# Attention by pairs of heads with shared half tiles, one rounding of query and key together, and straight-line code

## The chip, the cores and the metric
The kernel runs on one core of a Trainium2 chip. The metric is the device time of one launch in microseconds, median of several runs. The core's engines work at the same time, each through its own instruction list, and wait for one another on semaphores: TensorE (PE; PEld are its weight loads), VectorE (DVE), ScalarE (ACT), GpSimd (POOL) and SyncE (SP), which here issues nearly all DMAs. SBUF is the on-chip memory of 128 partitions; matrix results land in PSUM.

## The reference
```python
def _attn_ref(q, k, v):                     # q, k, v: 4 x 8 heads x 576 x 64
    ...
    def rotate(x):
        x1, x2 = (x[..., :half], x[..., half:])
        return np.concatenate([x1 * cos - x2 * sin, x1 * sin + x2 * cos], axis=-1)
    q_rot, k_rot = (rotate(q), rotate(k))
    scores = scale * np.matmul(q_rot, k_rot.transpose(0, 1, 3, 2))
    scores = scores - np.max(scores, axis=-1, keepdims=True)
    attn = np.exp(scores)
    attn = attn / (np.sum(attn, axis=-1, keepdims=True) + 1e-09)
    return np.matmul(attn, v)

def _moe_ref(x, w_in, w_out, s, b):         # 2304 x 512, weights 512 x 2048 and 2048 x 512
    r = np.maximum(x @ w_in, 0.0)
    return (s * (r * r) + b) @ w_out

def _moe2_ref(x, w_in, w_out):
    h = x @ w_in
    return (h * (1.0 / (1.0 + np.exp(-1.702 * h)))) @ w_out
```
The output is `_moe2_ref(_moe_ref(attention, heads side by side))`, in float32.

## The kernel before
Accurate products are built of rounded ones: a float32 value is split in a high part (type fp32r) and a low part, the rest, and a product takes two or three fp32r matmuls. Transposes are float32 matmuls against the identity `id_sb`.

Attention works head by head, 32 heads of 576 rows, that is four tiles of 128 and one half tile of 64. The jobs of a head: GpSimd rotates q and k (`rotate`, L348; VectorE for head 0). TensorE transposes both together (`prep`, L520). ScalarE rounds q and k (`hi_q`, `hi_k`), VectorE makes the low parts (`lo_q`, `lo_k`), each on 64 partitions, and SP copies the two parts of K to the other 64 partitions (`copy_halves`, L388). A score job (`S_job`, L476) makes 128 rows of scores by 576 keys in four matmuls (256 and 320 columns, with K's high and low part); VectorE takes the maximum of a row (L595), ScalarE the exp with its sum (L542). A transpose job (`X_job`, L487) turns one block column of E: four transposes of 128 rows and one of 64. ScalarE rounds the result (L549), VectorE subtracts (L602), and `PV` (L496) multiplies by V, high and low part side by side, in 18 matmuls. ScalarE takes the result out of PSUM in two halves (`main_out`, `rest_out`), GpSimd adds these per pair of heads; the inverse sums are widened, transposed (`B_job`, L510), and VectorE multiplies (`finish`, L613) into `xT`.

Each engine follows an order written by hand, a list of tokens such as `S2@1`: job S, tile 2, of the head one ahead (`PE_ORDER`, L229, and the lists behind it). `steps` (L284) unrolls the first and last heads and runs the rest as a loop over pairs. `SLOTS` says which of four PSUM tiles of two banks a job uses; a job waits until its predecessor in the tile has been read (`released`, L253).

The two MLPs follow in six chunks of 384 tokens each. In a step i of 16, `H` (L720) makes 128 hidden rows (12 matmuls), ScalarE and VectorE apply the function and split it, and `Y` (L736) adds the products of step i - 2 to the output. Weights come by DMA, are split by both engines, and stay in SBUF; four of them are split before the MLP begins. The first and last chunk of each MLP are unrolled, the others a loop of two chunks (`chunks`, L683).

## Time and profile before
| | us |
|---|---|
| median of 3 runs | 1200.91 (1199.67 to 1201.15) |
| span of the profiled execution | 1201.6 |
| TensorE busy | 1157.1 |
| VectorE busy | 596.4 |
| ScalarE busy | 584.1 |
| GpSimd busy | 218.5 |

The profile is of one execution; its span goes from the first to the last instruction. The first MLP's first matmul starts at 390.54 us, so attention takes about a third of the span. The chain that ended last is to 85% TensorE, 66% of it the two lines of the MLP (L732 and L756).

### The profile page before, as it was taken

To read this page: it belongs to the slowest core of one execution; us is meant where nothing else is said; L and a number is where in the kernel's file an instruction comes from. 1 tells how busy PE (TensorE), PEld (TensorE's weight loads), DVE (VectorE), ACT (ScalarE), POOL (GpSimd) and SP (SyncE) were. 2 spreads that over 40 slices of the span, in tenths; PEclk is the share of its full clock that TensorE was granted. 3 is DMA by queue.
4 is the path that set the end of the run, shared out by engine and by line. 5 is a ranking of instruction groups with operands and counts; after the bars stand their busy time and mean duration, and the time that the engine had idled before them with its cause. 6 is when DMAs were issued, how large, how long until landed. Compare 5 with 4: busy or idle time off the path is not lost.

```text
span 1201.6 us, 19306 instructions
## 1 busy us (share of the span) xinstructions
PE 1157.1 (96%) x6576; PEld 1054.0 (88%) x6576; DVE 596.4 (50%) x954; ACT 584.1 (49%) x1146; POOL 218.5 (18%) x310
## 2 busy tenths in 40 slices
PE   3999999999998999999999999999999999999998
PEld 3777887787786999999899999999999999999997
DVE  3788888888886653333233334653332322323222
ACT  3888989989986543323222234542222222223222
POOL 5466576566541000000000000000000000000000
PEclk9999999999998999999999999999999999999999
DMA  4322232232230430000000001320000000000000
GB/s 112 83 67 65 71 75 58 68 75 65 65 86 18 130 99 2 1 1 1 2 1 1 1 1 53 123 71 1 27 1 1 27 1 26 0 26 0 27 1 27
DMA packets 66437, 46.78 MB, mean 39 GB/s; under 512 B 30672, under 2 KB 55888, under 8 KB 66384
## 3 DMA queue, kind: packets, MB, share of 16 engines
q1 hardware_dynamic: 66384, 46.03, 14.0%
q8 instruction: 38, 0.62, 0.2%
q14 instruction: 15, 0.12, 0.0%
HBM read 31.85 MB, written 4.72 MB: 30 GB/s over the span
## 4 chain that ended last, share of the span: by engine, by line
PE 85%; ACT 7%; issue 5%; DVE 2%; DMA 0%; SPq 0%; ACTq 0%; DVEq 0%
PE hps L732 33%; PE acc L756 33%; PE psum L506 7%; PE psum L483 4%; ACT E L542 4%; PE psum L493 4%; PE psum L530 2%; ACT out_rest L563 1%; ACT EThi L549 1%; PE psum L517 1%; DVE ETlo L602 1%; DVE negmax L595 1%; ACTq L43 0%; DMA Klo<-Klo 0%; DMA kraw<-in_k_dram 0%
## 5 line engine op out<-in xcount | busy, mean ns | idle before, releaser
L732 PE MATMUL hps<-xlo,Whi 128*128 128x384 f32 x768 | 257.3, 335 | 1.8 <-issue 1.8
L732 PE MATMUL hps<-xhi,Whi 128*128 128x384 f32 x768 | 257.9, 336 | 0.6 <-issue 0.6
L732 PE MATMUL hps<-xhi,Wlo 128*128 128x384 f32 x768 | 257.8, 336 | 0.0
L732 PEld LDWEIGHTS hps<-xlo,Whi 128*128 128x128 f32 x768 | 144.2, 188 | 6.2 <-issue 2.2
L732 PEld LDWEIGHTS hps<-xhi,Whi 128*128 128x128 f32 x768 | 144.4, 188 | 5.2 <-issue 0.9
L732 PEld LDWEIGHTS hps<-xhi,Wlo 128*128 128x128 f32 x768 | 144.1, 188 | 0.0
L493 PE MATMUL psum<-id_sb,E 128*128 128x128 f32 (+1 forms) x800 | 134.1, 280 | 9.9 <-ACT E L542 7.2
L595 DVE TENSOR_REDUCE negmax<-psum 128x1 f32<-128x576 f32 (+1 forms) x160 | 120.4, 754 | 42.3 <-PE psum L483 41.1
L493 PEld LDWEIGHTS psum<-id_sb,E 128*128 128x128 f32 (+1 forms) x800 | 97.2, 141 | 49.5 <-issue 27.4
L834 ACT ACTIVATE ghi<-act,sb_sb 128x384 fp32r<-128x384 f32 x96 | 59.2, 617 | 157.8 <-PE acc L756 149.5
L858 DVE SCALAR_TENSOR_TENSOR glo<-act,sb_sb,ghi 128x384 fp32r<-128x384 f32 x96 | 59.5, 619 | 145.9 <-ACT ghi L834 145.9
L756 PE MATMUL acc<-ghi,Wlo 128*128 128x384 f32 x384 | 129.0, 336 | 0.0
L861 DVE TENSOR_TENSOR glo<-act,ghi 128x384 fp32r<-128x384 f32 x96 | 53.6, 559 | 151.7 <-ACT ghi L836 151.7
L756 PE MATMUL acc<-glo,Whi 128*128 128x384 f32 x384 | 128.9, 336 | 0.0
L756 PE MATMUL acc<-ghi,Whi 128*128 128x384 f32 x384 | 128.8, 335 | 0.0
L542 ACT ACTIVATE E<-psum,negmax 128x576 f32<-128x576 f32 (+1 forms) x160 | 119.0, 744 | 16.8 <-DVE negmax L595 16.3
L836 ACT CAST ghi<-act 128x384 fp32r<-128x384 f32 x96 | 49.3, 514 | 156.7 <-PE acc L756 156.7
L483 PE MATMUL psum<-Khi,Q 128*128 128x256 f32 x320 | 104.7, 348 | 12.6 <-ACT E L542 8.8
L855 DVE TENSOR_TENSOR act<-hps,act 128x384 f32<-128x384 f32 x96 | 53.5, 558 | 124.1 <-ACT act L830 124.1
L756 PE MATMUL acc<-Wlo,ghi 128*128 128x512 f32 x288 | 113.9, 396 | 0.0
L756 PE MATMUL acc<-Whi,glo 128*128 128x512 f32 x288 | 113.7, 395 | 0.0
L756 PE MATMUL acc<-Whi,ghi 128*128 128x512 f32 x288 | 111.9, 389 | 0.0
(66 smaller groups left out, 1897.4 us busy)
## 6 DMA issues: line engine op xcount, KB each, us to landing
wraw<-in_moe_w_in_dram SPq DMA_DIRECT2D x32, 256.0 KB, 2.7
wraw<-in_moe_w_out_dram SPq DMA_DIRECT2D x32, 256.0 KB, 3.0
Khi<-Khi SPq DMA_DIRECT2D x32, 144.0 KB, 2.3
Klo<-Klo SPq DMA_DIRECT2D x32, 144.0 KB, 2.5
out_dram<-xT SPq DMA_DIRECT2D x6, 768.0 KB, 3.5
qraw<-in_q_dram SPq DMA_DIRECT2D x32, 128.0 KB, 2.2
kraw<-in_k_dram SPq DMA_DIRECT2D x32, 128.0 KB, 2.2
vraw<-in_v_dram SPq DMA_DIRECT2D x32, 128.0 KB, 2.0
```

The lines of the kernel that those rows point to most:

```text
L483: mm = pe.matmul(ps[:, C0 + a:C0 + b], Q[h.odd][:, j * P:(j + 1) * P], K[h.odd][:, a:b], start=(n == 0), stop=(n == 1))
L493: mm = pe.transpose(ps[:, a:b], E[h.odd][0:rows, t, j * P:(j + 1) * P], id_sb[0:rows, 0:rows])
L506: mm = pe.matmul(O[:, C0 + a:C0 + b], V[h.odd][:, j, :, :].rearrange("p a d -> p (a d)"), X[:, j, a:b], start=(j == 0 and n == 0), stop=(j ...
L542: act.activation(E[h.odd][0:rows, j, 0:S], row(psum_of(h, "S", j))[0:rows], ACT.Exp, bias=negmax[h.odd][0:rows, j:j + 1], accum_out=sums[h ...
L595: dve.tensor_reduce(negmax[h.odd][0:rows, j:j + 1], row(psum_of(h, "S", j))[0:rows], AX_X, ALU.max, negate=True).then_inc(max_done, 1)
L732: mm = pe.matmul(ps[:, 0:CH], w[i][:, kt * P:(kt + 1) * P], piece(x[par][:], kt), start=(kt == 0 and j == 0), stop=(kt == KT - 1 and j == 2))
L756: mm = pe.matmul(dst, lhsT, rhs, start=(i == 0 and j == 0), stop=(i == NF - 1 and j == 2))
L834: act.activation(ghi[i % 2][:], a[:], ACT.Identity, bias=sb_sb[:, 1:2]).then_inc(g_hi, 1)
L836: act.copy(ghi[i % 2][:], a[:]).then_inc(g_hi, 1)
L855: dve.tensor_tensor(a[:], hps[i % HB][:, 0:CH], a[:], ALU.mult).then_inc(g_done, 1)
L858: dve.scalar_tensor_tensor(glo[i % 2][:], a[:], sb_sb[:, 1:2], ghi[i % 2][:].bitcast(F32), ALU.add, ALU.subtract).then_inc(g_lo, 1)
L861: dve.tensor_tensor(glo[i % 2][:], a[:], ghi[i % 2][:].bitcast(F32), ALU.subtract).then_inc(g_lo, 1)
```

## The change
Attention now works pair by pair. E's half tiles of the two heads share tiles: for the second head of a pair the tokens are laid out so that its half tile comes first, and one score job (`ST`) makes the 64 tail rows of both heads at once, in ten matmuls; one transpose job (`XT`) makes both heads' tail columns. All transposes have 128 rows and 128 columns. `PV` takes 20 matmuls. Query and key are rotated in one set of instructions over both, rounded in one instruction with a scale per partition, and the low part is one instruction too; four DMAs then copy Q's parts and K's parts to their places. ScalarE copies the result of `PV` once, whole (`evac`), and a DMA brings the half that is needed on the other partitions (`load_rest`). V's high part moves from ScalarE to GpSimd, the widening of the inverse sums from ScalarE to VectorE, and `finish` has three instructions. k and v are loaded in the layout that q had. All engines' lists are straight code: a static order for 16 pairs (`program`), also for GpSimd and SP, and the MLP's loops are unrolled in the same order of steps. One weight tile is split early and two at the end of attention; each chunk's output leaves in six DMAs where one did.

```diff
-    PE_ORDER = order("X0@0 S2@1 X1@0 S3@1 X2@0 S4@1 X3@0 X4@0 "
-                     "prep@3 S0@2 PV0@0 PV1@0 B@-1 PV2@0 PV3@0 PV4@0 S1@2")
+PE_ORDER = order("PV0@-1 B@-2 X00@0 prep1@1 X01@0 X02@0 S00@1 X03@0 PV1@-1 S01@1 S02@1 X10@0 X11@0 ST@1 prep0@2 "
+                 "XT@0 S03@1 S10@1 X12@0 S11@1 X13@0 S12@1 S13@1")
+POOL_ORDER = order("add0@-2 vlo1@-1 add1@-2 V0@0 vlo0@0 rot0@2 V1@0 rot1@2")
+SP_ORDER = order("load1@0 loadv0@-1 rest1@-3 load0@1 copy0@0 copy1@0 loadv1@-1 rest0@-2")
...
+def program(toks, ops, after=None):
+    for s in range(FIRST, NPAIR + 4):
+        for kind, h, j, ahead in toks:
+            if 0 <= s + ahead < NPAIR:
+                ops[kind](s + ahead, h, j)
+        if after:
+            after(s)
...
-    def steps(eng, order, ops, after=None):
-        with eng.Fori(lo // 2, hi // 2) as pair:
-            for odd in range(2):
-                step(Head(pair, odd))
...
-    def rotate(eng, h, n, by_cos, by_sin, chain, done, before):
-        for t, by in ((cos, by_cos), (sin, by_sin)):
-            eng.tensor_tensor(by[:, :, :].rearrange("p t (a f) -> p t a f", a=2), halves,
-                              tabs[t][:, :, :].unsqueeze(2).broadcast_to([P, NT, 2, HALF]), ALU.mult).then_inc(chain, 1)
+    def rotate(eng, g, by_cos, by_sin, chain, done, count):
+        for tab, by in ((cos, by_cos), (sin, by_sin)):
+            eng.tensor_tensor(by.rearrange("p t w (a f) -> p t (w a) f", a=2), halves,
+                              tab[:, :, :].unsqueeze(2).broadcast_to([P, NT, 4, HALF]), ALU.mult).then_inc(chain, 1)
...
-        def copy_halves(h):
-            e, g = h.odd, h.g
-            need(sp, k_hi, g + 1)
-            sp.dma_start(Khi[e][0:D, :].bitcast(F32), Khi[e][D:P, :].bitcast(F32)).then_inc(copied[e], 16)
-            need(sp, k_lo, g + 1)
-            sp.dma_start(Klo[e][0:D, :].bitcast(F32), Klo[e][D:P, :].bitcast(F32)).then_inc(copied[e], 16)
+        def copies(p, h, _):
+            sp.wait_ge(qk_lo, 2 * p + h + 1)
+            need(sp, s_done, 2 * NM * (p - 1) + NM * (h + 1))
+            need(sp, sT_done, p)
+            at = h * TAIL
+            for part in range(2):
+                sp.dma_start(Q[h][rows_of(part), at:at + S].bitcast(F32), QK[h][0:D, part, :].bitcast(F32)).then_inc(copied[h], 16)
+            for half in range(2):
+                sp.dma_start(K[h][rows_of(half), :, :].bitcast(F32), QK[h][D:P, :, :].bitcast(F32)).then_inc(copied[h], 16)
...
+        def load_rest(p, h, _):
+            sp.wait_ge(evac_done, 2 * p + h + 1)
+            need(sp, added, 2 * (p - 1) + h + 1)
+            sp.dma_start(rest[rows_of(h), :], O[h][rows_of(1 - h), :]).then_inc(rest_in[h], 16)
...
+        def hi_V(p, h, _):
+            pool.wait_ge(v_in[h], 32 * (p + 1))
+            need(pool, pv_done, 2 * (p - 1) + h + 1)
+            pool.tensor_tensor(V[h][:, :, h, :], vraw[h][:], zero[:, :].unsqueeze(2).broadcast_to([P, NT, D]), ALU.add).then_inc(v_hi, 1)
...
+        def add(p, h, _):
+            pool.wait_ge(evac_done, 2 * p + h + 1)
+            pool.wait_ge(rest_in[h], 16 * (p + 1))
+            need(pool, x_done, p)
+            r = rows_of(h)
+            if h == 0:
+                pool.tensor_tensor(osum[r, :], O[0][r, :], rest[r, :], ALU.add).then_inc(added, 1)
+            else:
+                for signal in made:
+                    pool.wait_ge(signal, made[signal])
+                pool.tensor_tensor(osum[r, 0:MAIN], O[1][r, TAIL:S], rest[r, TAIL:S], ALU.add)
+                pool.tensor_tensor(osum[r, MAIN:S], O[1][r, 0:TAIL], rest[r, 0:TAIL], ALU.add).then_inc(added, 1)
...
-            for a, b in HALVES:
-                for n, K in enumerate((Khi, Klo)):
-                    mm = pe.matmul(ps[:, C0 + a:C0 + b], Q[h.odd][:, j * P:(j + 1) * P], K[h.odd][:, a:b],
-                                   start=(n == 0), stop=(n == 1))
+            for a, b, c in PIECES[h]:
+                for part in range(2):
+                    mm = pe.matmul(ps[:, a:b], Q[h][:, at:at + P], K[h][:, part, c:c + b - a], start=part == 0, stop=part == 1)
+        def ST_job(p, _, __):
+            for h in range(2):
+                pe.wait_ge(copied[h], 64 * (p + 1))
+            freed(pe, before[("ST", p, 0, 0)])
+            ps, r = banks("ST"), ROW[0]
+            tails = Q[0][:, MAIN:MAIN + P], Q[1][:, 0:P]
+            for a, b, parts in ((r, BANK, ((0, r, 0, BANK - r), (1, r, TAIL, TAIL + BANK - r))),
+                                (BANK, r + S, ((0, BANK, BANK - r, S), (1, BANK, TAIL + BANK - r, S), (1, r + MAIN, 0, TAIL)))):
+                for n, (h, at, c, d) in enumerate(parts):
+                    for part in range(2):
+                        mm = pe.matmul(ps[:, at:at + d - c], tails[h], K[h][:, part, c:d], start=n == 0 and part == 0,
+                                       stop=n == len(parts) - 1 and part == 1, skip_group_check=True)
+            mm.then_inc(sT_done, 1)
...
-            for t in range(NT):
-                rows = P if t < NT - 1 else TAIL
-                a, b = cols(t)
-                mm = pe.transpose(ps[:, a:b], E[h.odd][0:rows, t, j * P:(j + 1) * P], id_sb[0:rows, 0:rows])
+            ps, r = banks("X", h, j), ROW[0]
+            at = r + MAIN if h == 0 else r - P
+            pe.transpose(ps[:, at:at + P], ET[p % 2][:, j * P:(j + 1) * P], id_sb[:])
+            c = h * TAIL + j * P
+            for t in range(NM):
+                mm = pe.transpose(ps[:, r + t * P:r + (t + 1) * P], E[p % 2][:, t, h, c:c + P], id_sb[:])
+        def XT_job(p, _, __):
+            pe.wait_ge(exp_done, 2 * NM * (p + 1))
+            pe.wait_ge(expT_done, p + 1)
+            freed(pe, before[("XT", p, 0, 0)])
+            ps, r = banks("XT"), ROW[0]
+            pe.transpose(ps[:, r - P:r], ET[p % 2][:, S - P:S], id_sb[:])
+            pe.transpose(ps[:, r + MAIN:r + MAIN + P], ET[p % 2][:, MAIN:MAIN + P], id_sb[:])
+            for t in range(NM):
+                both = E[p % 2][:, t, :, :].rearrange("p h s -> p (h s)")[:, MAIN:MAIN + P]
...
-            for a, b in HALVES:
-                parts = (EThi, ETlo) if j < NT - 1 else (EThi,)
-                for n, X in enumerate(parts):
-                    mm = pe.matmul(O[:, C0 + a:C0 + b], V[h.odd][:, j, :, :].rearrange("p a d -> p (a d)"), X[:, j, a:b],
-                                   start=(j == 0 and n == 0), stop=(j == NT - 1))
+            shift = TAIL if h == 0 else 0
+            for j in range(NT):
+                for a, b, c in PIECES[h]:
+                    for n in range(2):
+                        if j < NM:
+                            x = (Xhi, Xlo)[n][h][:, j, c:c + b - a]
+                        else:
+                            x = (XThi, XTlo)[n][:, c + shift:c + shift + b - a]
+                        mm = pe.matmul(ps[:, a:b], V[h][:, j, :, :].rearrange("p a d -> p (a d)"), x,
+                                       start=j == 0 and n == 0, stop=j == NM and n == 1)
+            mm.then_inc(pv_done, 1)
...
-        def main_out(h, _):
-            need(act, pv_done, NT * (h.g + 1))
-            need(act, x_done, h.pair)
-            act.copy(out_main[mine(h), :], psum_of(h, "PV")[mine(h), C0:C0 + S]).then_inc(main_done, 1)
-        def rest_out(h, _):
-            need(act, pv_done, NT * (h.g + 1))
-            need(act, added, h.pair)
-            act.copy(out_rest[mine(h), :], psum_of(h, "PV")[mine(h + 1), C0:C0 + S]).then_inc(rest_done, 1)
+        def evac(p, h, _):
+            act.wait_ge(pv_done, 2 * p + h + 1)
+            need(act, added, 2 * (p - 1) + h + 1)
+            act.copy(O[h][:], row(banks("PV", h), h)).then_inc(evac_done, 1)
-        def hi_q(h, _):
-            need(act, prep_t, h.g + 1)
-            need(act, s_done, NT * (h.g - 1))
-            act.activation(Q[h.odd][0:D, 0:S], row(psum_of(h, "prep"))[0:D], ACT.Copy, scale=SCALE).then_inc(q_hi, 1)
-        def hi_k(h, _):
-            need(act, prep_t, h.g + 1)
-            need(act, s_done, NT * (h.g - 1))
-            act.copy(Khi[h.odd][D:P, :], row(psum_of(h, "prep"))[D:P]).then_inc(k_hi, 1)
+        def qk(p, h, _):
+            act.wait_ge(prep_t, 2 * p + h + 1)
+            need(act, copied[h], 64 * p)
+            act.activation(QK[h][:, 0, :], row(banks("prep", h), h), ACT.Identity, scale=qk_scale[:, 0:1]).then_inc(qk_hi, 1)
-        def lo_k(h, _):
-            need(dve, k_hi, h.g + 1)
-            dve.tensor_tensor(Klo[h.odd][D:P, :], row(psum_of(h, "prep"))[D:P], Khi[h.odd][D:P, :].bitcast(F32),
-                              ALU.subtract).then_inc(k_lo, 1)
+        def qk_low(p, h, _):
+            dve.wait_ge(qk_hi, 2 * p + h + 1)
+            dve.scalar_tensor_tensor(QK[h][:, 1, :], row(banks("prep", h), h), qk_scale[:, 0:1],
+                                     QK[h][:, 0, :].bitcast(F32), ALU.mult, ALU.subtract).then_inc(qk_lo, 1)
...
+            dve.reciprocal(inv_c[:], sums_eps[:]).then_inc(inv_step, 1)
+            dve.wait_ge(inv_step, p + 1)
+            dve.tensor_copy(inv[:], inv_c[:, 0:2 * NM].rearrange("p (h t) -> p t h", h=2).unsqueeze(3)
+                            .broadcast_to([P, NM, 2, D])).then_inc(inv_done, 1)
+        def finish_pair(p):
+            b, t = p // KT * S, p % KT
+            ps, r = banks("B"), ROW[0]
+            dve.wait_ge(b_done, p + 1)
+            dve.wait_ge(added, 2 * p + 2)
+            dve.tensor_tensor(xT[:, t, b:b + MAIN], ps[:, r:r + MAIN], osum[:, 0:MAIN], ALU.mult)
+            for h in range(2):
+                at = r + MAIN + h * TAIL
+                last = dve.tensor_tensor(xT[rows_of(h), t, b + MAIN:b + S], ps[rows_of(h), at:at + TAIL],
+                                         osum[rows_of(h), MAIN:S], ALU.mult)
+            last.then_inc(x_done, 1)
...
+    if s == NPAIR - 1:
+        eng.wait_ge(prep_t, 2 * NPAIR)
+        eng.wait_ge(v_lo, 2 * NPAIR)
+        for i in range(EARLY, AHEAD):
+            split_w(eng, i, hi)
...
-def chunks(eng, chunk):
-    for mlp in range(2):
-        first = mlp * NCH
-        chunk(first, 0, mlp)
-        with eng.Fori(0, (NCH - 2) // 2) as two:
-            for o in range(2):
-                chunk(2 * two + (first + 1 + o), (1 + o) % 2, mlp)
-        chunk(first + NCH - 1, (NCH - 1) % 2, mlp)
+        for n in range(STEPS + LAG):
+            if n < STEPS:
+                H_step(pe, n)
+            if n >= LAG:
+                Y_step(pe, n - LAG)
```

Here is TensorE's list in the loop of attention before, from the end of one score job to the next; L493 is a transpose job of E, L530 the transposes of q and k, L483 a score job, L506 `PV`:
```order
L483 MATMUL psum<-Klo,Q 128x320
L493 MATMUL psum<-id_sb,E 128x128 x4
L493 MATMUL psum<-id_sb,E 128x64
L493 MATMUL psum<-id_sb,E 128x128 x4
L493 MATMUL psum<-id_sb,E 128x64
L530 MATMUL psum<-id_sb,qkrot 128x128 x4
L530 MATMUL psum<-id_sb,qkrot 128x64
L483 MATMUL psum<-Khi,Q 128x256
L483 MATMUL psum<-Klo,Q 128x256
```
And after the change the same kind of place, behind the first `PV` of a step (L482), with the transpose jobs of E and ET (L448 and L451), those of q and k (L502 and L504) and a score job (L424):
```order
L482 MATMUL psum<-XThi,V 128x320
L482 MATMUL psum<-XTlo,V 128x320
L448 MATMUL psum<-id_sb,ET 128x128
L451 MATMUL psum<-id_sb,E 128x128 x4
L502 MATMUL psum<-id_sb,rot 128x128
L504 MATMUL psum<-id_sb,rot 128x128 x4
L448 MATMUL psum<-id_sb,ET 128x128
L451 MATMUL psum<-id_sb,E 128x128 x4
L448 MATMUL psum<-id_sb,ET 128x128
L451 MATMUL psum<-id_sb,E 128x128 x4
L424 MATMUL psum<-K,Q 128x256 x2
L424 MATMUL psum<-K,Q 128x320 x2
```
A job of one head still has five transposes, and none of them has 64 rows or columns now.

SP's queue in the loop before, for one head: the loads of q and k, the two copies of K, the load of V.
```order
L365 DMA qraw<-in_q_dram 128x4x64
L366 ISA
L366 DMA qraw<-in_q_dram 64x64
L370 DMA kraw<-in_k_dram 128x256
L371 DMA kraw<-in_k_dram 64x64
L43 REGISTER_ALU
L391 DMA Khi<-Khi 64x576
L393 DMA Klo<-Klo 64x576
L384 DMA vraw<-in_v_dram 128x256
L386 DMA vraw<-in_v_dram 64x64 x2
```
After, for the latter part of a pair (`QK` holds both rounded parts, `O` the copied result of `PV`):
```order
L329 DMA Q<-QK 64x576 x2
L331 DMA K<-QK 64x1152 x2
L329 DMA Q<-QK 64x576 x2
L331 DMA K<-QK 64x1152 x2
L320 DMA vraw<-in_v_dram 128x4x64
L321 DMA vraw<-in_v_dram 64x64
L336 DMA rest<-O 64x576
```
Four copies a head stand where two stood, and the V load of the second head stands behind all of them.

GpSimd's list before, for the first head of a pair and the rotation of the next: rotation (L354 to L360), V's low part (L447).
```order
L354 TENSOR_TENSOR byc<-kraw,kc 128x320
L354 TENSOR_TENSOR bys<-kraw,ks 128x320
L43 REGISTER_ALU
L359 TENSOR_TENSOR qkrot<-byc,bys 128x5x32
L360 TENSOR_TENSOR qkrot<-bys,byc 128x5x32
L43 ISA
L447 TENSOR_TENSOR V<-vraw,V 128x5x64
```
After, from the rounding of the second head's V on (L385 high part, L390 low part, L400 to L406 the sums of a pair):
```order
L385 TENSOR_TENSOR V<-vraw,zero 128x5x64
L301 TENSOR_TENSOR byc<-raw,cos 128x640
L301 TENSOR_TENSOR bys<-raw,sin 128x640
L306 TENSOR_TENSOR rot<-byc,bys 128x10x32
L307 TENSOR_TENSOR rot<-bys,byc 128x10x32
L400 TENSOR_TENSOR osum<-O,rest 64x576
L390 TENSOR_TENSOR V<-vraw,V 128x5x64
L405 TENSOR_TENSOR osum<-O,rest 64x512
L406 TENSOR_TENSOR osum<-O,rest 64x64
```
The rotation has half as many instructions of twice the size, V's high part is new here, and the sums stand between two rotations.

## Rows read from the trace of the kernel before

**Rows 1.** The page: busy times, and TensorE's busy tenths in 40 slices
```profile
PE 1157.1 (96%) x6576; PEld 1054.0 (88%) x6576; DVE 596.4 (50%) x954; ACT 584.1 (49%) x1146; POOL 218.5 (18%) x310
PE   3999999999998999999999999999999999999998
```
**Rows 2.** Stretches: us, busy PE PEld DVE ACT POOL (instructions), clock, DMA, GB/s
```profile
60.00:346.00 286.00, 274.45 (x1816) 225.46 (x1816) 240.00 (x375) 256.64 (x527) 180.76 (x247) 1.00 0.28 68
...
376.00:383.00 7.00, 4.89 (x33) 3.64 (x31) 3.97 (x8) 3.19 (x5) 0.00 (x0) 1.00 0.00 1
383.00:391.00 8.00, 7.61 (x33) 6.63 (x33) 2.91 (x4) 4.17 (x7) 0.00 (x0) 0.57 0.21 67
...
396.00:398.00 2.00, 2.00 (x14) 2.00 (x13) 1.68 (x3) 0.98 (x2) 0.00 (x0) 1.00 0.73 245
...
591.00:596.00 5.00, 5.00 (x22) 5.00 (x21) 0.82 (x2) 1.11 (x2) 0.00 (x0) 0.66 0.01 3
```
**Rows 3.** Timeline of TensorE: start, us, instruction; broadcasts L517, first MLP matmul L732
```profile
65.38 0.80 PE L517 MATMUL psum<-id_sb,invb 128*128 128x128 f32 x5
...
353.81 0.80 PE L517 MATMUL psum<-id_sb,invb 128*128 128x128 f32 x5
...
390.54 0.44 PE L732 MATMUL hps<-xhi,Whi 128*128 128x384 f32 x1
```
**Rows 4.** Timeline of TensorE: score and transpose jobs, a 64-row load
```profile
289.68 0.29 PE L483 MATMUL psum<-Khi,Q 128*128 128x256 f32 x1
289.81 0.28 PE L483 MATMUL psum<-Klo,Q 128*128 128x256 f32 x1
...
290.22 0.80 PE L493 MATMUL psum<-id_sb,E 128*128 128x128 f32 x5
290.95 0.39 PE L483 MATMUL psum<-Khi,Q 128*128 128x256 f32 x1
...
291.59 0.60 PE L493 MATMUL psum<-id_sb,E 128*128 128x128 f32 x4
...
350.55 0.66 PE L493 MATMUL psum<-id_sb,E 128*128 128x128 f32 x4 [0.17 <-ACT E L542]
351.14 0.13 PEld L493 LDWEIGHTS psum<-id_sb,E 64*128 64x128 f32 x1 [0.17 <-issue]
```
**Rows 5.** Groups by shape, 60 to 346 us: busy, mean ns, idle before
```profile
L493 PEld LDWEIGHTS psum<-id_sb,E 64*128 64x128 f32 x128 | 17.2, 135 | 21.4 <-issue 21.4
```
**Rows 6.** The chain that ended last, in order of time: start, us
```profile
320.27 2.38 PE psum L506 x18
...
397.05 2.08 PE acc L756 x12
```
**Rows 7.** Groups by shape, 60 to 346 us, on the other engines
```profile
L595 DVE TENSOR_REDUCE negmax<-psum 128x1 f32<-128x576 f32 x103 | 77.8, 756 | 16.4 <-PE psum L483 15.5
...
L542 ACT ACTIVATE E<-psum,negmax 128x576 f32<-128x576 f32 x102 | 76.1, 746 | 7.9 <-DVE negmax L595 7.5
...
L549 ACT CAST EThi<-psum 128x576 fp32r<-128x576 f32 x102 | 65.3, 641 | 3.1
...
L354 POOL TENSOR_TENSOR byc<-qraw,qc 128x320 f32<-128x320 f32 x26 | 22.6, 867 | 0.0
...
L452 POOL TENSOR_TENSOR out_main<-out_main,out_rest 128x576 f32<-128x576 f32 x13 | 18.3, 1410 | 0.0
```
**Rows 8.** DMA issues of the whole span: count, KB each, median us to landing
```profile
wraw<-in_moe_w_out_dram SPq DMA_DIRECT2D x32, 256.0 KB, 3.0
Khi<-Khi SPq DMA_DIRECT2D x32, 144.0 KB, 2.3
```
**Rows 9.** Timeline near the start: an issue on SP, a matmul of a score job
```profile
15.12 0.49 SPq L391 DMA_DIRECT2D Khi<-Khi  x1
...
18.72 0.41 PE L483 MATMUL psum<-Klo,Q 128*128 128x256 f32 x1
```
**Rows 10.** Timeline of TensorE at the loop's back jump in the first MLP
```profile
586.97 0.44 PE L732 MATMUL hps<-xhi,Whi 128*128 128x384 f32 x1 [0.63 <-issue]
...
590.29 0.45 PE L732 MATMUL hps<-xlo,Whi 128*128 128x384 f32 x1 [1.85 <-issue]
```

988 lines of the change are left out of this document (471 added, 517 removed).

## Prediction
> **What bounds the kernel now.** I read the page first. TensorE is busy for 96% of the span, VectorE and ScalarE for half, and TensorE's digit is 9 in nearly all of the 40 slices [rows 1]. So the time is TensorE's; an edit pays only by its matmuls, its waits or its clock. Next the table of stretches. In steady attention (60 to 346 us) TensorE is busy 274.5 of 286 us, ScalarE 256.6, VectorE 240.0 and GpSimd 180.8, at a granted clock of 1.00 [rows 2]. The broadcast transposes of pair 0 and pair 13 start at 65.38 and 353.81 us [rows 3]: 288.4 us for 13 pairs, 22.2 us a pair, of which 21.3 are TensorE work (96% [rows 2]) and 0.9 waits. The MLP runs from 390.54 us [rows 3] to the end, 811.1 us.
>
> What a reader should find is what these 21.3 us consist of. A score job (four matmuls, 1152 columns) after another kind of matmul takes 0.54 us (289.68 to 290.22). A transpose job (four of 128x128, one of 64 rows) takes 0.73 us (290.22 to 290.95), and the score job behind it 0.64 us (290.95 to 291.59) [rows 4]. Four full transposes start within 0.39 us (0.66 less the 0.27 that the last one lasts), a first one of 0.17 after a wait and 0.11 for each further one; the 64-row weight load waits 0.17 us though nothing holds it [rows 4]. The profile counts 128 such loads in steady attention with 21.4 us of waits [rows 5]. So the half tile, with half the rows, costs 0.73 + 0.10 (the longer score job) - 4 x 0.11 = 0.39 us, some 0.40, where a full one costs 0.11.
>
> The Trainium skill ("TensorEngine Tiling (Array Packing)", Key Properties) says that changing the tiling mode drains TensorE. By that rule all of the stall goes wherever the stationary tiles have 128 rows, 4.2 us a pair in the sum below; without it the part behind the job could stay, and the sum would be 0.8.
>
> The rows put the wait in front of the 64-row load itself; what comes behind the job, 0.28 us with the longer score job, could also be the end of a transpose job of any shape. That reading is a rival below.
>
> **TensorE, per pair.** Before there are 13 transpose jobs a pair (10 of E, 2 of q/k, 1 of the sums), each with one 64-row transpose: 13 x (4 x 0.11 + 0.40) = 10.9 us. Now there are 40 + 6 + 10 + 5 = 61 transposes, all 128x128: 6.7 us. That takes 4.2 off. Scores: ten jobs of 0.54 become eight plus the shared tail job, ten matmuls with 2304 columns, which I put at 1.15 from the 0.54 of two 256- and two 320-column matmuls [rows 4] (twice that, and two of 64 columns): +0.1. PV: 18 matmuls in 2.38 us [rows 6] become 20, +0.27 a head, +0.5 a pair. Sum: 21.3 - 4.2 + 0.1 + 0.5 = 17.7 us. No row shows a full transpose followed by a matmul; between 0 and 0.1 us in each of six places, I take 0 for all, since a matmul to transpose change adds nothing.
>
> **The other engines, per pair** [rows 7]. ScalarE: nine exps at 0.75 with some 0.1 of their accumulator read uncovered, nine roundings at 0.64, two merged q/k roundings and two copies of PV at 0.65: 16 us, from 19.9. VectorE: nine maxima and nine subtractions at 0.75, two merged lows 0.75, the inversion with its new 512-element copy about 1, the product in three pieces about 1.1: 17 us, from 18.5. Both fit below 17.7, barely; I don't count them as bound. GpSimd: an instruction of 320 elements lasts 0.87, of 576 1.41, so about 2.1 ns an element; the merged rotation (two of 640, two of 320) is then 2 x 1.55 + 2 x 0.87 = 4.8 us a head, V's rounding and rest 4 x 0.88, the sums 1.41 + 1.6: 16.2 us, from 13.9.
>
> **What is late next.** Before, a head's K copies were 288 KB, two DMAs. Now Q and K are both rounded as one tile and copied by four DMAs of 144, 144, 288 and 288 KB, issued one behind the other on SP at some 0.5 us each [rows 9]. A 144 KB copy lands after 2.3 us [rows 8], and the fastest stretch I found moves 245 GB/s [rows 2]: 2.3 + 0.74 MB / 245 GB/s = 5.3 us from the low part to the last copy landed. Two chains hang on it.
> (a) Within TensorE's order: prep of the second head (position 4), its rounding 0.65 and low part 0.75 with handovers, 5.3 us of copies: 7.0 us until the shared tail score job may start. TensorE has X01, X02, S00, X03, PV1, S01, S02, X10, X11 in between: 4 x 0.55 + 3 x 0.54 + 2.65 = 6.5 us. It waits 0.5 us or more.
> (b) Around the pair: V of the second head is rounded on GpSimd (0.9), then its rotation (4.8), the two sums and V's low part (1.4 + 0.9 + 1.6), then the product on VectorE (1.1), one subtraction and the low part of q/k (1.5), then SP issues four copies and only behind them the next V load, whose data comes behind theirs (5.3 + 0.6), and the next V is rounded. 18.1 us, and some ten handovers at about 0.1: 19.1 us for one pair. This circle is longer than TensorE's 17.7. Behind VectorE's wait for the sum stand the subtractions that free the PSUM tiles, so TensorE feels it.
> The four PSUM tiles add short waits behind exps, as now (0.9 us a pair). I take 19.3 us a pair; bounds 18.3 (only TensorE's work and waits like today's) and 21 (GpSimd's longer instructions twice their present length, copies at half that rate).
>
> **Start, end of attention, MLP.** Start: one rotation instead of two, yet four copies instead of two, and 9 score jobs of pair 0 before its first transpose; the matmuls there still take 0.41 us instead of 0.28 until about 39 us [rows 9, 4]. Pair 0's broadcast comes at about 67 us, 1.6 later; bounds -3 and +6. Then 13 pairs: 288.4 - 13 x 19.3 = 37.5 us gained. From pair 13's broadcast to the MLP 36.7 us pass now [rows 3]; in there TensorE idles 2.1 us in 376 to 383, and its mean clock is 0.57 from 383 to 391 [rows 2], because the last head is worked off alone. After: the rest of a step without scores (9 transpose jobs, PV of two heads) some 12, two more PV and two broadcasts 6.4, waits 1.5, since ScalarE's weight roundings now wait for V's last low part in front of hi10 to hiT, and a slow clock 1.5: 21.4 us. Gain 15.3.
> MLP: same matmuls. In the loop version a gap of 0.63 and 1.85 us without a releaser stands at the loop's back jump in the first MLP, and the clock is halved some 3.4 us after it [rows 10, 2]: 2.5 + 1.7 = 4.2 us that straight-line code should not have. Weights: three are split before the MLP instead of four; each later one has a step of 4.16 us (24 matmuls, 2 x 2.08 [rows 6]) for its load (its second half lands 3.0 us after its issue [rows 8]) and two roundings, and two of them are under way at a time, so I cost it at 1 us at the entry. Output: six smaller DMAs a chunk; only the last chunk counts, five more issues at 0.4 to 0.5, of which smaller pieces give back some: +1.7. Net gain 1.5.
>
> The Trainium skill ("Runtime: NRT & Kernel Launch", Instruction fetch mechanics) says a taken branch outside the present window stalls until the target is fetched, and straight code is prefetched. By that rule every back jump would show a gap; the trace shows it at one back jump of the first MLP and none in the second, where TensorE's digits are 9 from 780 us to the last slice [rows 1]. So the sum takes only the one gap measured; by the rule it would be about the same.
>
> **Sum.** -1.6 + 37.5 + 15.3 + 1.5 = 52.7 us. The profiled span is 1201.6 us, 0.7 over the median of 1200.91. 1201.6 - 52.7 - 0.7 = 1148 us.
>
> **Rivals.** (R1) The forecast, 1148. (R2) The circle or the copies cost more: 20.5 to 21 us a pair, 13 x 1.5 = 20 us later: 1168. For it: GpSimd at 16 of 19 us and 22 DMA issues a pair on SP (11 us). Against: each single price lies near a row. (R3) The stall belongs to the end of a transpose job, not to 64 rows: TensorE keeps about 0.28 us in 12 jobs, 3.4 us, 21.1 with waits 22.0 a pair; only the ends gain: 1148 + 13 x 2.7 = 1183. Against: the wait stands in front of the 64-row load itself [rows 4]. (R4) Copies and V loads overlap better than the 245 GB/s bound and the chains fall behind TensorE: 18.3 a pair, 1135. (R5) Slower than before: TensorE's wait for the copies, now at one place of each pair, lets the clock fall to 1.2 GHz in the loop. Half-clock work costs its own length once more, so it decides from 52.7 us lost: 105 us at half clock, 8 us a pair (of 22); at 12 us a pair the time would be 1148 + 13 x 6 = 1226. For it: at 383 us the clock fell after TensorE had been busy 4.9 of 7 us [rows 2]. Against: the loop of before with 0.9 us idle in 22 held 1.00 throughout.
>
> The Trainium skill ("TensorE: Matmul & The Clock Gate", Part 4: PE-mode transpose) says transposes do not count as busy for the clock gate. It speaks for R5 at the end of attention, where nearly only transposes run, and against it in the loop, where their share falls from 10.9 of 22 to 6.7 of 19 us; the trace of before holds the full clock even at that larger share, so the rule changes the chance of R5 little.
>
> **Numbers.** R1 0.55, R2 0.2, R4 0.13, R3 0.07, R5 0.04, code fetch or something unnamed 0.01. The time is R1's. The range goes from R4 less some at the ends, 1130, to R2 with a late start, 1176: about 0.85 of the chance. 0.2% is 2.4 us, about what a measurement tells from none. Faster 0.95, same 0.01, slower 0.04.
>
> **What would show it.** Right: no 0.17 us stall before transposes, transposes at 0.11, a score job behind them at 0.54, TensorE's work 17.7 and a pair 19.3 us; its longest wait before the shared tail job, on a DMA; GpSimd waiting for V's DMA once a pair; no gap at 586 us. Wrong: score jobs still 0.64 behind full transposes (R3), a granted clock under 1 in the loop (R5), VectorE or ScalarE without waits, which would make them the bound, or a pair under 18 us.

## The result, and the profile after

The changed kernel takes 1187.8 us (median of 4 runs, 1185.22 to 1190.36) against 1201.03 of the kernel before; the ratio is 0.989, 95% interval 0.987 to 0.991. It is faster by 1.1%, clear of the noise: 13 us where 53 were forecast, and 1187.8 lies above the range of 1130 to 1176 us. In the runs further down, one of four of e4 (1575.7 us) and one of the kernel before (3828.8 us) fell in a slow state and are left out, so all times and ratios are of fast runs.

The page after: busy times, then tenths in 40 slices.
```profile
PE 1127.1 (95%) x6608; PEld 1056.7 (89%) x6608; DVE 571.4 (48%) x910; ACT 508.2 (43%) x999; POOL 250.9 (21%) x250
PE   4888999898998999999999999999999999999997
```
The matmuls' busy time is 30.0 us shorter [rows 1], the span 13.0: more than half of what left TensorE came back as waits. The slices of attention (the first 13) now hold many eights.

The timeline of TensorE after: broadcasts of pair 0 and of pair 13, first MLP matmul.
```profile
74.53 0.27 PE L491 MATMUL psum<-id_sb,inv_c 128*128 128x128 f32 x1
...
358.23 0.27 PE L491 MATMUL psum<-id_sb,inv_c 128*128 128x128 f32 x1
...
381.26 0.42 PE L683 MATMUL psum<-xhi,Whi 128*128 128x384 f32 x1
```
These answer to [rows 3] and split the miss of 39.8 us (all but 0.2 of it):

| stretch | forecast | after | late by |
|---|---|---|---|
| pair 0's broadcast at | 67.0 | 74.5 | 7.5 |
| 13 pairs | 250.9 (19.3 each) | 283.7 (21.8 each) | 32.8 |
| pair 13's broadcast to the MLP | 21.4 | 23.0 | 1.6 |
| MLP to the end | 809.6 | 807.3 | -2.3 |

Stretches after (columns as in [rows 2]): steady attention, the end of attention, and where the back jump was.
```profile
100.00:350.00 250.00, 227.27 (x1638) 203.90 (x1639) 200.27 (x307) 173.34 (x357) 177.88 (x168) 0.99 0.63 137
358.20:381.30 23.10, 17.46 (x124) 16.81 (x122) 11.22 (x22) 9.64 (x15) 6.34 (x8) 0.85 0.09 20
574.00:586.00 12.00, 12.00 (x71) 12.00 (x70) 3.33 (x6) 3.26 (x7) 0.00 (x0) 1.00 0.00 0
```
TensorE is busy 91% in the loop (96% before); no engine is full. The third row has no gap, where [rows 10] had 2.5 us and a halved clock.

Transposes (timeline), and their weight loads, 100 to 350 us (group by shape).
```profile
251.94 0.27 PE L448 MATMUL psum<-id_sb,ET 128*128 128x128 f32 x1
252.05 0.60 PE L451 MATMUL psum<-id_sb,E 128*128 128x128 f32 x4
252.49 0.27 PE L502 MATMUL psum<-id_sb,rot 128*128 128x128 f32 x1
...
L451 PEld LDWEIGHTS psum<-id_sb,E 128*128 128x128 f32 x368 | 43.0, 140 | 0.1
```
A job of five transposes takes 0.55 us (251.94 to 252.49), and 368 weight loads wait 0.1 us together; in [rows 5] 128 waited 21.4. TensorE's work fell as forecast. So where did the time go? First the waits (whole run), then SP and GpSimd in one pair (timeline).
```profile
POOL byc L301 <- DMA raw<-in_k_dram: 55.0, 17, 11.2
POOL V L385 <- DMA vraw<-in_v_dram: 46.9, 14, 7.7
```
```profile
255.16 1.10 SPq L329 DMA_DIRECT2D Q<-QK  x2
256.30 1.25 SPq L331 DMA_DIRECT2D K<-QK  x2
257.59 0.76 SPq L320 DMA_DIRECT2D vraw<-in_v_dram  x1
258.40 1.54 SPq L321 DMA_DIRECT2D vraw<-in_v_dram  x1
260.03 0.55 SPq L336 DMA_DIRECT2D rest<-O  x1
260.63 0.59 SPq L314 DMA_DIRECT2D raw<-in_q_dram  x1
...
262.51 0.52 SPq L315 DMA_DIRECT2D raw<-in_k_dram  x1
```
```profile
247.54 0.88 POOL L307 TENSOR_TENSOR rot<-bys,byc 128x320 f32<-128x320 f32 x1
...
261.92 0.72 POOL L385 TENSOR_TENSOR V<-vraw,zero 128x320 fp32r<-128x320 f32 x1 [2.70 <-DMA vraw<-in_v_dram]
264.70 1.56 POOL L301 TENSOR_TENSOR byc<-raw,cos 128x640 f32<-128x640 f32 x1 [2.06 <-DMA raw<-in_k_dram]
```
GpSimd waits twice a pair. The first wait (V behind the copies) is in the forecast circle; the second is not: the q and k loads of the second head stand in SP's order behind copies, V load and `rest` load, although the rotation that read their tile had ended at 248.4. V was rounded at 262.64 and the rotation began at 264.70, so the circle closes through the q and k loads, and V's wait stands beside it with 2.1 us to spare. What hangs on it is VectorE's product, in the chain of waits:
```profile
252.13 0.33 POOL osum L406
...
252.56 0.69 DVE xT L601
...
253.65 0.76 DVE Xlo L574
```
Behind it stand the subtractions that free score tiles, as the prediction said.

### The profile page after: what moved, and what is told of

The parts are those of the page before. It is cut to its first block, busy times and chain, and to the rows that moved or that the text cites. A ratio compares the mean times of both kernels' runs of the same rounds, so it can differ in the third digit from the quotient of the medians.

```text
span 1188.6 us, 17369 instructions
## 1 busy us (share of the span) xinstructions
PE 1127.1 (95%) x6608; PEld 1056.7 (89%) x6608; DVE 571.4 (48%) x910; ACT 508.2 (43%) x999; POOL 250.9 (21%) x250
## 4 chain that ended last, share of the span: by engine, by line
PE 73%; DVE 2%; ACT 1%; issue 1%; POOL 0%; DMA 0%; SPq 0%; ACTq 0%; DVEq 0%; POOLq 0%
PE psum L683 34%; PE psum L711 34%; PE psum L482 2%; PE psum L424 1%; PE psum L451 1%; DVE Xlo L574 1%; DVE negmax L564 1%; PE psum L438 0%; ACT Xhi L533 0%; ACT E L520 0%; DMA K<-QK 0%; PE psum L448 0%; PE psum L494 0%; ACT QK L548 0%; DVE QK L610 0%
## 5 line engine op out<-in xcount | busy, mean ns | idle before, releaser
L683 PE MATMUL psum<-xhi,Wlo 128*128 128x384 f32 x768 | 257.8, 336 | 0.0
L683 PE MATMUL psum<-xhi,Whi 128*128 128x384 f32 x768 | 257.6, 335 | 0.0
L683 PE MATMUL psum<-xlo,Whi 128*128 128x384 f32 x768 | 257.2, 335 | 0.0
L683 PEld LDWEIGHTS psum<-xhi,Whi 128*128 128x128 f32 x768 | 144.2, 188 | 4.2
L683 PEld LDWEIGHTS psum<-xlo,Whi 128*128 128x128 f32 x768 | 144.2, 188 | 4.1
L683 PEld LDWEIGHTS psum<-xhi,Wlo 128*128 128x128 f32 x768 | 144.1, 188 | 0.0
L711 PE MATMUL psum<-ghi,Whi 128*128 128x384 f32 x384 | 128.3, 334 | 0.0
L711 PE MATMUL psum<-glo,Whi 128*128 128x384 f32 x384 | 128.3, 334 | 0.0
L711 PE MATMUL psum<-ghi,Wlo 128*128 128x384 f32 x384 | 128.3, 334 | 0.0
L424 PE MATMUL psum<-K,Q 128*128 128x320 f32 (+1 forms) x512 | 100.6, 327 | 27.4 <-DVE Xlo L574 10.2
L424 PEld LDWEIGHTS psum<-K,Q 128*128 128x128 f32 x512 | 75.3, 197 | 48.4 <-issue 15.8
L711 PE MATMUL psum<-Wlo,ghi 128*128 128x512 f32 x288 | 113.9, 396 | 0.0
```

The source lines that it names most:

```text
L424: mm = pe.matmul(ps[:, a:b], Q[h][:, at:at + P], K[h][:, part, c:c + b - a], start=part == 0, stop=part == 1)
L683: mm = pe.matmul(hps(n), w[i][:, kt * P:(kt + 1) * P], x[C % 2][:, kt, :], start=kt == 0 and j == 0, stop=kt == KT - 1 and j == 2)
L711: mm = pe.matmul(dst, lhsT, rhs, start=i == 0 and j == 0, stop=i == NF - 1 and j == 2)
```

## The experiments

Each was timed beside the kernel before. Start is pair 0's broadcast, pair the mean of the 13 pairs from there to pair 13's, both from one profile of each kernel; the MLP takes 807.3 to 807.4 us in every variant of the changed kernel.

| run | us | ratio (95%) | start | pair |
|---|---|---|---|---|
| changed kernel | 1187.8 | 0.989 (0.987-0.991) | 74.5 | 21.82 |
| e1_raw_first | 1182.7 | 0.985 (0.983-0.987) | 76.1 | 21.06 |
| e2_raw_v_first | 1176.5 | 0.980 (0.979-0.982) | 76.4 | 20.64 |
| e3_before_full_tiles | 1180.5 | 0.983 (0.981-0.985) | 61.8 | 21.03 |
| e4_half_k_copies | 1176.9 | 0.979 (0.976-0.982) | 71.0 | 21.03 |
| e5_weights_later | 1177.2 | 0.981 (0.980-0.983) | 76.4 | 20.61 |
| e6_widen_on_scalar | 1175.6 | 0.980 (0.978-0.981) | 75.4 | 20.58 |
| e7_both | 1175.5 | 0.979 (0.978-0.981) | 75.4 | 20.61 |
| e8_copy_twice | 1188.5 | 0.990 (0.989-0.992) | 77.3 | 21.48 |
| e9_widen_half_k | 1172.2 | 0.978 (0.976-0.979) | 71.1 | 20.61 |
| e10_round_early | 1185.2 | 0.988 (0.986-0.990) | 78.2 | 21.15 |
| e11_early_half_k | 1181.8 | 0.985 (0.983-0.987) | 73.5 | 21.14 |
| e12_short_broadcast | 1174.2 | 0.979 (0.977-0.981) | 76.7 | 20.46 |
| e13_half_maximum | 1170.3 | 0.976 (0.974-0.978) | 72.4 | 20.33 |
| e14_half_max_half_k | 1160.9 | 0.967 (0.964-0.970) | 68.3 | 19.98 |

### SyncE's queue
```diff
-    SP_ORDER = order("load1@0 loadv0@-1 rest1@-3 load0@1 copy0@0 copy1@0 loadv1@-1 rest0@-2")
+e1  SP_ORDER = order("loadv0@-1 rest1@-3 load0@1 copy0@0 load1@1 copy1@0 loadv1@-1 rest0@-2")
+e2  SP_ORDER = order("loadv0@-1 rest1@-3 load0@1 copy0@0 load1@1 loadv1@-1 copy1@0 rest0@-2")
```


> One edit: in SP's order the q/k load of a pair's second head stands in front of the copies of that head's rotated q and k instead of behind them, the V load and the rest load. Theory A (one circle per pair through GpSimd, VectorE's product and SP's queue sets 21.8 us a pair): GpSimd's wait for raw k, 2.06 us between V's rounding and the rotation, goes, and a pair falls to about 19.7 us, the time to about 1158. Rival B (TensorE's own work, 19.9 us busy, and the four PSUM tiles set the pair): less than 0.5 us a pair, 1181 or more. Rival C (the copies' DMA traffic, 0.63 of the DMA engines, sets it): no change, 1188.

> As the first, and the V load of the second head too stands in front of the copies. Theory A: GpSimd never waits for a load that stands behind the copies; the circle is broken, and what is next is TensorE with its wait for the copies before the shared tail job: about 19.3 us a pair, 1150 us. Rival B: 21 us a pair or more, 1178 or more. Rival C: 21.8, 1188.

The q/k loads alone brought 0.76 us a pair, V's with them 1.18: less than theory A has it (19.7 and 19.3 us a pair) and more than rival B (under 0.5 us, and 21 us a pair or more). So a circle was there, and another bound stands close behind it. In the waits of e2, 100 to 340 us, GpSimd waits for no DMA any more, but for PV, which reads V's only buffer:
```profile
POOL V L385 <- PE psum L482: 53.5, 23, 5.2
```
The circle is gone; 20.64 us a pair remain, far from TensorE's 17.7. e2 leaves nothing out and beats both kernels; so do e5, e6 and e7, within 1.0 us of it.

### The half tile's stall, alone
```diff
-                        rows = P if t < NT - 1 else TAIL
-                        mm = pe.transpose(ps[:, a:b], E[h.odd][0:rows, t, j * P:(j + 1) * P], id_sb[0:rows, 0:rows])
+                        mm = pe.transpose(ps[:, a:a + P], E[h.odd][:, t, j * P:(j + 1) * P], id_sb[:])
```
The same in the other two transposes, on the kernel before; E's unused rows are zeroed once.

> The kernel before with only this changed: the 64-row transposes take 128 rows (E's unused rows are zeroed once), so 13 more rows-of-64 a pair are transposed but the tile shape never changes. Theory (the half tile costs 0.39 us because its shape changes, 0.28 more than a full one): TensorE's work falls from 21.3 by 3.6 us a pair, ScalarE with 19.9 us becomes the bound, about 20.5 us a pair, 1177 us. Rival (the cost belongs to the end of every transpose job): 0 to 0.1 us a job, within 0.5 us a pair of 22.1, 1193 or more.

The timeline of e3: a transpose job and the score job behind it.
```profile
201.29 0.71 PE L493 MATMUL psum<-id_sb,E 128*128 128x128 f32 x5
201.76 0.36 PE L484 MATMUL psum<-Khi,Q 128*128 128x256 f32 x1
201.96 0.28 PE L484 MATMUL psum<-Klo,Q 128*128 128x256 f32 x1
```
The transposes take 0.47 us for 0.73 [rows 4], so the stall is that of the 64-row tile, and R3 falls. Behind the job nothing is lost either: the second score matmul starts 0.20 us after the first, where 0.12 is usual, but the first starts only 0.03 us after the last transpose (201.29 + 0.71 - 0.27 = 201.73), where 0.11 is usual, and both ways the sum is 0.23. The Trainium skill ("TensorEngine Tiling (Array Packing)", Key Properties) has a change of tiling mode drain TensorE; the run agrees in so far as 0.26 us less are spent in a job with one mode. Yet 13 such savings, 3.4 us or somewhat more, moved the pair from 22.2 to 21.0 only, where 20.5 was expected: in 100 to 340 us ScalarE is busy 222 of 240.
```profile
100.00:340.00 240.00, 221.57 (x1622) 196.57 (x1620) 214.42 (x334) 222.25 (x471) 155.18 (x211) 1.00 0.30 72
```
This one part brings more than the whole change.

### Half of the K copies
```diff
-                    for half in range(2):
+                    for half in range(1):
                         sp.dma_start(K[h][rows_of(half), :, :].bitcast(F32), QK[h][D:P, :, :].bitcast(F32)).then_inc(copied[h], 16)
```
on the changed kernel; the other 64 rows of K are zero.

> The changed kernel without the second of the two copies of K per head (288 KB; those rows of K stay zero, so Q's low part is left out of the scores). Theory A: SP's issues behind it come 0.62 us earlier and the V load is not behind 288 KB, so the circle shortens by 0.6 to 1.8 us: 20 to 21.2 us a pair, 1165 to 1180. Rival B: under 0.3 us a pair. Rival C (bandwidth): the copies' traffic falls by a third, a pair falls by 2 us or more, the most of these kernels.

0.79 us less a pair, as much as e1, and 3.5 us less at the start. That is within theory A. Rival C (the copies' bandwidth) falls: it asked for 2 us or more, and in e9 below the same halving moves the pair not at all.

### Weights later, the widening copy on ScalarE, both, and the copy twice
```diff
 e5, e7 (on e2)
-                    if s in (0, 1, 8):
+                    if s in (3, 4, 8):
 e6, e7 (on e2), with ACT_ORDER "exp00@0 wide@-2 evac1@-2 ..."
-                    dve.tensor_copy(inv[:], inv_c[:, 0:2 * NM]...)
+                def widen(p, _, __):
+                    act.wait_ge(inv_step, p + 1)
+                    act.copy(inv[:], inv_c[:, 0:2 * NM]...).then_inc(inv_done, 1)
 e8 (on e2)
+                    dve.tensor_copy(inv2[:], inv_c[:, 0:2 * NM]...)
```


> The kernel of e2_raw_v_first (SyncE asks for raw tiles and V ahead of the copies; 1176.5 us, 20.64 us a pair, pair 0's broadcast at 76.4 us), with the first two weight transfers of the MLP asked for after steps 3 and 4 instead of 0 and 1, and the first weight split two steps later. Theory A, SyncE's queue sets the start: the two weight transfers (2.4 us of issue each, 1 MB each) stand at 20.26 and 41.83 us ahead of the q and k loads of the next pair; without them pair 0's broadcast comes 4 to 7 us earlier (70 to 72 us) and the time is 1170 to 1173 us at the same 20.6 us a pair. Theory B, the start is set by the new order (each step's scores wait for the K copies of the step's second head, 4.2 us of transfer behind its rotation, rounding and copies) and not by the weights: broadcast at 75 to 77, 1175 to 1178 us.

> The kernel of e2_raw_v_first with the widening copy of the reciprocals (128 x 512, 0.88 us on VectorE) made by ScalarE, ahead of its second eviction. Theory A, VectorE's chain with four score tiles paces the pair (the three inversion instructions take 1.5 us between two subtractions that free tiles, and TensorE's score job of the second head waits 0.60 us for VectorE): 0.6 to 1.0 us less a pair, 19.7 to 20.0, so 1164 to 1169 us. Theory B, TensorE's own work and the order of tiles pace the pair and VectorE has 3 us of slack: 20.5 to 20.7 a pair, 1175 to 1178 us. Theory C, ScalarE's evictions come later by the copy's 0.5 to 0.9 us and the chain through the evicted halves, GpSimd's sums and the finish pays for it: 21.0 to 21.4 a pair, 1181 to 1187 us.

> Both edits of e5_weights_later and e6_widen_on_scalar on e2_raw_v_first. If start and pair are separate terms the two differences add up, to within 1 us: 1159 to 1166 us if both theories A hold, 1170 to 1173 if only the start's does, 1164 to 1169 if only VectorE's does, 1175 to 1178 if neither.

> The kernel of e2_raw_v_first with VectorE's widening copy (0.88 us) made twice, the first into a tile that nothing reads. It asks for VectorE's slack from the other side. Theory A, VectorE's chain paces the pair: 0.7 to 0.95 us more a pair, 21.4 to 21.6, 1186 to 1189 us. Theory B, TensorE paces it and VectorE's 3 us of idle time in a pair can take the copy: 20.6 to 20.8 a pair, 1175 to 1179 us. Between the two if the copy stands at a place with some slack of its own.

The weights do nothing (start 76.4 both times), my theory A for the start falls (and a weight is two DMAs of 256 KB, not the 1 MB that I wrote). VectorE's copy gave 0.06 us a pair when it left, so theory B held there, and took 0.84 when doubled, so theory A held there: VectorE's chain and something else were nearly tied. What else stood there the chain of waits of e6 shows:
```profile
239.65 0.45 PE psum L451 x4
...
240.13 0.65 ACT Xhi L533
...
240.80 0.76 DVE Xlo L579
241.56 0.74 DVE QK L612
...
242.31 0.48 SPq L329
...
244.14 4.09 DMA K<-QK
...
248.32 1.39 PE psum L438 x10
```
TensorE's tail scores wait for the K copies, the prediction's chain (a), and from one such job (228.09) to the next (248.32) it is 20.2 us. Such a closed chain, which comes back to the same job one pair later, is called a ring here.

### Half copies again, earlier rounding
e9 is e4's edit on e6; e10 moves, on e6, the second rounding ahead of the broadcast; e11 is both.
```diff
-    PE_ORDER = order("PV0@-1 B@-2 X00@0 prep1@1 X01@0 ...
+    PE_ORDER = order("PV0@-1 prep1@1 X00@0 B@-2 X01@0 ...
-    ACT_ORDER  ... evac0@-1 hi00@0 qk1@1 hi01@0 ...        DVE_ORDER  ... finish@-2 lo00@0 klo1@1 lo01@0 ...
+    ACT_ORDER  ... evac0@-1 qk1@1 hi00@0 hi01@0 ...        DVE_ORDER  ... klo1@1 lo00@0 finish@-2 lo01@0 ...
```


> The kernel of e6_widen_on_scalar (20.58 us a pair, 1175.6 us) without the second of the two K copies of each head; its 64 rows of K stay zero, so the scores come from half of the products. It leaves one issue (0.6 us) and one transfer (median landing 4.0 us with two copies, 3.4 with one) out of every chain from rounding to scores, and 25 of 142 GB/s. Theory A, with VectorE relieved the pair is a ring through the copies: the tail scores (1.39 us) wait for the K copies, release the next rounding, the last scores, PV, the second rounding and the next copies, 20.2 us round in the chain of e6: it shrinks by 1.2 to 2 us until the next bound, TensorE's own 19.1 us: 19.2 to 19.9 a pair, 1158 to 1168 us. Theory B, the pair is TensorE's work and the waits of its score jobs for free tiles (0.60 us each for VectorE's rounding, which the copies don't touch): 20.3 to 20.6, 1171 to 1176 us.

> The kernel of e6_widen_on_scalar with the second rounding of a pair straight behind PV and the broadcast two jobs later (on TensorE, ScalarE and VectorE; the two jobs exchange their score tiles). Nothing is left out. In the ring of theory A this takes one transpose job (0.55 us) and part of a rounding (0.65 us on ScalarE, 0.76 on VectorE) out of the way between PV and the copies: 0.6 to 1.2 us less a pair, 19.4 to 20.0, 1161 to 1168 us. Theory B (free tiles and TensorE): the broadcast now waits for the eviction of PV's tile (0.65 us) and nothing gets shorter: 20.5 to 21.0, 1175 to 1181 us.

> Both edits of e9_widen_half_k and e10_round_early, with half of the K rows left zero as in the first of them. It asks what bounds the pair once the ring is shorter twice. If the ring is what each shortens, the two gains do not add up: TensorE's own 19.1 us and its waits for free tiles stop them at 19.2 to 19.7 a pair, 1157 to 1163 us. If the start shortens with the ring as well (two rounds of it lie ahead of the first broadcast), 2 us less in pair 0's broadcast.

Theory A was wrong as put and B held: e9's pair is 20.61. Only its start is 4.3 us earlier. The chain of e9 has no DMA; a maximum and an exp hold the tile that the tail scores want, and rounding, maximum and exp stand behind them:
```profile
242.56 0.55 PE psum L424 x4
243.14 0.77 DVE negmax L569
...
244.57 0.20 ACT E L520
...
244.91 1.39 PE psum L438 x10
```
From 224.73 to 244.91 it is again 20.2 us. e10 was worse than both theories, 0.57 us more a pair: in its chain VectorE's product now stands behind two subtractions (its last part starts at 228.14) and holds the broadcast's tile, which the transpose job X03 needs (228.52). e11, forecast at 19.2 to 19.7, shows the same with fewer copies.

### Less TensorE work, shorter holds, and both rings at once
```diff
 e12 (on e6): four of the five transposes of B_job left out
-                        mm = pe.transpose(ps[:, r + t * P:r + (t + 1) * P], both, id_sb[:])
 e13 (on e6), and the same for the tail
-                    dve.tensor_reduce(negmax[p % 2][:, c:c + 1], row(banks("S", h, j), h), AX_X, ...
+                    dve.tensor_reduce(negmax[p % 2][:, c:c + 1], row(banks("S", h, j), h)[:, 0:S // 2], AX_X, ...
```
e14 is e13 with e9's edit.

> The kernel of e6_widen_on_scalar (20.58 us a pair, 1175.6 us) with four of the five transposes of the broadcast left out, 0.436 us of TensorE's own work a pair, and nothing else; the main columns of the broadcast keep what the tile held. Theory A, what is left of the pair is one ring through TensorE's jobs in their order and the holding times of the four score tiles (rounding or maximum, then exponential, then the next job in that tile), and the broadcast stands on it between PV and the transposes: 0.3 to 0.45 us less a pair, 20.15 to 20.3, 1169 to 1172 us. Theory B, the ring passes beside the broadcast (the tile of PV or the halves' sums decide there): 20.5 to 20.6, 1174 to 1177 us.

> The kernel of e6_widen_on_scalar with each maximum taken over 288 instead of 576 columns of its tile, on VectorE 0.75 us before and an estimated 0.4 to 0.5 now (the subtraction over 384 columns of 0.66 and of 640 of 0.81 us give the slope). TensorE's and ScalarE's instructions are the same. Theory A, score tiles are held too long, not TensorE's work: two maxima stand on the ring of tiles in the chain of e6 and of e9, so 0.5 to 0.8 us less a pair, 19.8 to 20.1, 1163 to 1168 us. Theory B, TensorE's work and its in-order jobs are the bound: 20.5 to 20.6 a pair, 1174 to 1177 us.

> Both edits of e13_half_maximum (20.33 us a pair) and e9_widen_half_k (20.61) on e6_widen_on_scalar (20.58): maxima over half of the columns, and half of the K rows left zero instead of copied. Theory A, several rings of nearly the same length stand side by side (the one through the K copies, 20.2 us round in the chains of e6, e12 and e13, and the one through the held score tiles, 20.2 in the chain of e9), so one shortened alone leaves the other: together they give clearly more than the sum of the two single gains (0.25 - 0.03 us), 19.0 to 19.8 a pair, and with the start's 4 us 1149 to 1160 us. Theory B, single gains add: 20.3 a pair, 1164 to 1168 us.

e12: 0.12 us less for 0.44 of work, between the theories. e13: the maximum takes 0.45 for 0.75 us, nine times a pair, and the pair loses 0.25, between the theories too. Each time the chain goes through the K copies (in e12 4.11 us from 244.86, then the tail job at 249.06; in e13 the round takes 19.8 us, 223.18 to 243.02, and not the 20.2 of my text on e14). e13 does not tell a tile held for less time from 2.7 us less work on VectorE.

e14 decides whether bounds are tied. Against e6, half copies alone change the pair by +0.03 us, half maxima alone by -0.25, both by -0.60, far more than the sum; the whole times say the same, 3.4 and 5.3 us less alone, 14.7 together. The bounds are tied, which is theory A; but the size is below the 0.8 to 1.6 us that it expected, so a third one lies not far below. In e14's waits of TensorE, 100 to 340 us, score tiles lead:
```profile
PE psum L424 <- DVE QK L612: 6.5, 11, 0.6
PE psum L424 <- ACT E L520: 4.6, 12, 0.4
PE psum L424 <- DVE Xlo L579: 3.4, 4, 1.1
```
The first of these is a score job whose tile VectorE's low part of q and k still reads; it costs 0.6 us once a pair in the changed kernel and in e2, e6, e9, e13 and e14 alike. That this third bound is the order of jobs over four tiles is the nearest reading and was not tried apart.

The mean of 13 pairs also hides that they are of four kinds. In e9, from broadcast to broadcast: seven of the first eight take 20.15 to 20.21 us, the third 23.1, the next four 20.9, the last 19.8. The first kind is what the edits move: 20.2 in e6 and e9, 19.9 in e13, 19.6 in e14. In the next four VectorE and ScalarE also split the first tokens for the MLP, and this stands in the chain, in e9 and in e13:
```profile
251.55 0.83 DVE xlo L223
```
```profile
249.05 1.39 DVE xlo L223
```
Such a pair is 20.9 us in e9, e13 and e14 alike, so no edit here moved that bound, and the forecast has no term for it; in the kernel before the same pairs take 22.1 like all others. The 23.1 is the pair in which the first weight is split: TensorE is busy 3.42 of 5 us (126 to 131), then the granted clock is 0.66 (131 to 135). Where the clock stays at 1.00 there, as in e2 and e6, that pair takes 21.6.

## Why the prediction was wrong

**TensorE's work, 17.7 us: right.** Transposes at 0.11 without stall, PV 2.65 us (248.75 to 251.40 in the timeline after; forecast 2.65), two score jobs in 1.07 (chain of e14; forecast 1.08). The tail job takes 1.22 to 1.32 us (240.68 to 242.00 is the longer) where I put 1.15. Behind a transpose nothing is lost where the next job needn't wait, as e3 showed, so taking 0 in six places was right. 61 x 0.11 + 2 x 2.65 + 8 x 0.53 + 1.3 is 17.5. The busy share says more, 227.27 of 250 us or 19.8 a pair, because a matmul in front of a wait counts as busy to its end (a transpose for 0.27 us, where the next starts 0.11 behind); of a pair of 21.8 us some 4 are waits, not 2.

**Circle (b), 19.1 us: this step failed.** It is 21.8 us. It went from V's rounding straight into "its rotation (4.8)", as if raw q and k were there; they came 2.06 us late, since I had followed the V load through SP's queue and not the five issues behind it (260.03 to 263.03). The copies with the V load cost 6.8 us from the low part's end (255.1) to V's rounding (261.92), not 5.9: with copies under way one issue took 1.54 us (258.40), where I had put 0.5. 19.1 + 2.1 + 0.9 = 22.1, near the 21.8 measured. e1 and e2 take these waits away: -1.18 us a pair.

**"The four PSUM tiles add short waits behind exps, as now (0.9 us a pair)": this failed too,** and costs as much. With the circle gone (e2) the pair stands at 20.6, 1.3 over the forecast, for 17.5 of work: 3.1 us of waits where 0.9 were put. e13 and e14 show two of the bounds that make them, the K copies and what VectorE's maxima cost, and that a third lies behind both; 0.2 to 0.3 us are the MLP's first split (four pairs 0.7 longer), which had no term. That the old stall hid the time for which tiles are held is my reading. e3 does not prove it: there 3.4 us of work gone gained 1.16, but ScalarE, busy 19.5 of 21.0 us, can be the bound.

**Chain (a), 7.0 us against 6.5: miscounted, and not the longest wait.** There are five transpose jobs in between (X01, X02, X03, X10, X11), not four, so the sum is 7.0 against 7.0. After the change the tail job waits for a DMA 0.5 us in all from 100 to 350 us; the longest waits are of score jobs for a subtraction (8.8). Only with the circle gone does the chain count, as one of the tied bounds at 20.2 us (e6: 3.6 us of such waits in 11 pairs).

**The other engines.** VectorE was put at 17 us, below the bound "barely": it is 17.5 (200.27 of 250), and e8 shows almost no slack in e2. The inversion, "about 1", is 1.98 us (means of 0.84, 0.22 and 0.92), see below.

**Start, 67 us: wrong by 7.5.** I put 1.6 us in all, for four copies against two and one rotation less. In the chain of e2's start the K copies stand three times before the first broadcast, at 4.2 us each:
```profile
19.61 4.17 DMA K<-QK
...
41.18 4.16 DMA K<-QK
...
61.31 4.33 DMA K<-QK
```
Halving them gives 3.5 to 4.7 us in all four pairs of runs (e4, e9, e11, e14); the weights give none. The rest stays open.

**End, 21.4 us: 23.0. MLP, 1.5 us gained: 3.8.** The back jump's 4.2 us are gone, TensorE waits nowhere at the entry (I had put 1), and the output's tail is 6.0 us for 5.0, 1.0 more where I had put 1.7. Why the end of attention took 1.6 us more wasn't looked into.

**The rivals.** R2 named the right mechanism at 1.2 to 1.7 us a pair; it is 2.5. R3's number was near the result for a wrong reason. R5 was wrong for the loop (clock 0.99), though the clock did fall once, behind the first weight's split: TensorE was busy 5.23 of 6 us (131 to 137), and the clock was 0.72 in the next six. In e9 and e7 that pair is 1.5 us longer than in e2.
